# Another order for the first loads, scans and splits of a gated scan feeding two feed-forward layers

## The reference

```
sig = 1 / (1 + exp(-f_logit));  f = lb + (1 - lb) * sig;  i = 1 - f
h = f[:, t] * h + i[:, t] * x[:, t];  y[:, t] = h          # t = 0 .. 6079
x1 = g1(y @ w_in0) @ w_out0       # g1(h) = h * sigmoid(1.702 * h)
z  = g2(x1 @ w_in1) @ w_out1      # g2(h) = 0 below -1, h above 1, (h + 1)^2 / 4 between
```

## Time and profile before

| | |
|---|---|
| median of three runs | 1020.7 us |
| the profiled execution | 1021.38 us |
| its span, first to last instruction | 1019.6 us |
| PE busy | 1009.2 us, 99% of the span |
| DVE, ACT, POOL busy | 67%, 69%, 57% |
| mean granted clock of PE, share of full | 0.998 |
| DMA | 130.76 MB, mean 128 GB/s; 277 and 235 GB/s in the first two slices of 25.5 us |

### The profile page before, as it was taken

The page is one execution under the profiler, slowest core; times in us unless marked ns, Lnnn a source line. Parts: engine busy times, 40 slices in busy tenths (PEclk is TensorE's granted clock), DMA queues, the critical chain, the costliest instruction groups (busy, mean ns, idle before and its releaser), DMA issues.

```text
span 1019.6 us, 14153 instructions
## 1 busy us (share of the span) xinstructions
PE 1009.2 (99%) x4401; PEld 823.6 (81%) x4401; DVE 686.8 (67%) x958; ACT 705.2 (69%) x1306; POOL 579.6 (57%) x471
## 2 busy tenths in 40 slices
PE   7999999999999999999999999999999999999998
PEld 5988988888888888888888888888888888888886
DVE  5864867675676786666678666668665456767676
ACT  6666767666676677667677676767766667777665
POOL 3567768757577465356636436645635664573432
PEclk9999999999999999999999999999999999999999
DMA  7776574435622222442322334232323223232421
GB/s 277 235 232 223 183 250 160 166 114 205 207 106 99 83 83 99 155 150 73 107 74 95 135 114 144 73 109 72 109 74 131 91 75 107 73 109 73 146 76 42
DMA packets 53212, 130.76 MB, mean 128 GB/s; under 512 B 6032, under 2 KB 16912, under 8 KB 52112
## 3 DMA queue, kind: packets, MB, share of 16 engines
q1 hardware_dynamic: 52992, 129.59, 36.5%
q10 hardware_dynamic: 144, 0.26, 0.1%
HBM read 106.82 MB, written 23.00 MB: 127 GB/s over the span
## 4 chain that ended last, share of the span: by engine, by line
PE 97%; ACT 1%; POOL 1%; DMA 0%; DVE 0%; issue 0%; SPq 0%; POOLq 0%; ACTq 0%
PE chain L561 26%; PE acc L616 17%; PE acc L613 17%; PE acc L612 17%; PE pair L561 13%; PE single L561 7%; DMA gate<-f_logit_dram 0%; POOL xin1lo L1415 0%; ACT g_hi L908 0%; DVE xin0lo L1143 0%; POOL w_main L1378 0%; SPq L489 0%; POOL g_lo L1441 0%; ACT g_act L894 0%; ACT xin0hi L795 0%
## 5 line engine op out<-in xcount | busy, mean ns | idle before, releaser
L1441 POOL TENSOR_TENSOR g_lo<-g_act,g_hi 128x512 fp32r<-128x512 f32 (+1 forms) x269 | 354.3, 1318 | 395.9 <-ACT g_hi L908 391.2
L868 ACT ACTIVATE spare<-chain 128x512 f32<-128x512 f32 x240 | 143.3, 597 | 189.8 <-PE chain L561 189.2
L1198 DVE TENSOR_TENSOR spare<-pair,spare 128x512 f32<-128x512 f32 x160 | 110.5, 691 | 182.3 <-PE pair L561 181.8
L908 ACT ACTIVATE g_hi<-g_act 128x512 fp32r<-128x512 f32 (+1 forms) x269 | 168.1, 625 | 5.5 <-DVE g_act L1222 3.4
L561 PE MATMUL chain<-xin1hi,w_main 128*128 128x512 f32 x416 | 162.5, 395 | 0.0
L616 PE MATMUL acc<-g_lo,w_down0hi 128*128 128x512 f32 (+1 forms) x384 | 150.3, 391 | 0.0
L612 PE MATMUL acc<-g_hi,w_down0hi 128*128 128x512 f32 (+1 forms) x384 | 149.8, 390 | 0.3 <-ACT g_hi L908 0.3
L616 PE MATMUL acc<-g_lo,w_down1hi 128*128 128x512 f32 (+1 forms) x384 | 150.1, 391 | 0.0
L613 PE MATMUL acc<-g_hi,w_down1lo 128*128 128x512 f32 (+1 forms) x384 | 150.0, 391 | 0.0
L613 PE MATMUL acc<-g_hi,w_down0lo 128*128 128x512 f32 (+1 forms) x384 | 150.0, 391 | 0.0
L612 PE MATMUL acc<-g_hi,w_down1hi 128*128 128x512 f32 (+1 forms) x384 | 149.7, 390 | 0.0
(11 more groups left out here) (125 smaller groups left out, 1966.1 us busy)
## 6 DMA issues: line engine op xcount, KB each, us to landing
w_main<-sums_kept SPq DMA_DIRECT2D x80, 512.0 KB, 3.6
w_main<-blocks_kept SPq DMA_DIRECT2D x80, 256.0 KB, 2.9
w_a<-blocks_kept SPq DMA_DIRECT2D x80, 128.0 KB, 3.9
blocks_kept<-w_main SPq DMA_DIRECT2D x16, 512.0 KB, 4.3
w_main<-blocks_kept SPq DMA_DIRECT2D x16, 512.0 KB, 3.4
sums_kept<-xin0hi SPq DMA_DIRECT2D x16, 512.0 KB, 2.9
zout<-w_in_dram SPq DMA_DIRECT2D x23, 256.0 KB, 4.3
out_dram<-zout SPq DMA_DIRECT2D x10, 512.0 KB, 5.5
```

Source lines behind the costliest of these rows:

```text
L868: act.activation(snap[k][:, 0:n], chain[g % 2][:, 0:n], ACT.Copy).then_inc(s_snap, 1)
L908: act.activation(g_hi[h % 4][:, 0:n], activated(h), ACT.Copy).then_inc(s_ghi, 1)
L1198: dve.tensor_tensor(to[:, 0:n], bank[:, 0:n], snap[(0, 2, 1)[k]][:, 0:n], ALU.add).then_inc(s_evac, 1)
L1441: pool.tensor_tensor(g_lo[h % 4][:, 0:n], g_act[h % 4][:, 0:n], g_hi[h % 4][:, 0:n].bitcast(F32), ALU.subtract).then_inc(s_glo_pool, 1)
```

## The change

- **First loads (SP and ACT).** The bound `lb` (1 KB) is issued by ACT and block 0 of the weights by SP. SP's order becomes gate part 0, gate part 1, first half of x, block 0, second half of the gate, block 1, second half of x; the rest stays.
- **Order on ACT.** `first_hi(0)` stands ahead of `sigmoid_step(0, 2)`; `first_hi(1)` ahead of `blocks_hi(0, 1)`; `f_step(0, 2)` behind both; `first_hi(2)` and `first_hi(3)` ahead of both `down_hi`.
- **Order on DVE.** Drive and scan of parts 0 and 1 run one after the other, then remainders 0 and 1; drive and scan of parts 2 and 3, then remainder 3.
- **One remainder on POOL.** Remainder 2 is made by POOL, after `blocks_lo(0, 1)` and ahead of `down_lo(0, 0)`. PE and SP wait for it on a semaphore of its own.
- **Next inputs.** `x_lo(1, 0)` moves from step 13 to step 11 of stage 0, waiting for `down_lo(0, 6)` instead of `down_lo(0, 7)`; `x_lo(1, 1)` moves from step 14 to 13 and waits for `down_lo(0, 7)`.

The number of matmuls, of compute instructions and of bytes moved stays the same.

```diff
-            load_first(gate, f_logit, part_columns(0, 0)[0], s_gate_first[0])
-            sp.dma_start(lb[:], lower_bound).then_inc(s_lb, 16)
+            for q in range(K):
+                load_first(gate, f_logit, part_columns(0, q)[0], s_gate_first[q])
             load_first(state, x, half(0), s_x_first[0])
-            load_first(gate, f_logit, part_columns(0, 1)[0], s_gate_first[1])
+            load_raw_up(0, 0)
+            load_first(gate, f_logit, half(1), s_gate_early[1])
             load_raw_up(0, 1)
-            load_first(gate, f_logit, half(1), s_gate_early[1])
             load_first(state, x, half(1), s_x_first[1])
...
                     for k in range(K):
-                        pe.wait_ge(s_first_lo, 2 * h + k + 1)
+                        if (h, k) == (1, 0):
+                            pe.wait_ge(s_first_lo_pool, 1)
+                        else:
+                            pe.wait_ge(s_first_lo, h + k + 1)
...
-            act.dma_start(raw_up[0], up_source[0][0]).then_inc(s_raw_up[0], 16)
+            act.dma_start(lb[:], lower_bound).then_inc(s_lb, 16)
             sigmoid_step(0, 0)
             sigmoid_step(0, 1)
             blocks_hi(0, 0)
+            first_hi(0)
             sigmoid_step(0, 2)
-            first_hi(0)
+            first_hi(1)
+            blocks_hi(0, 1)
             f_step(0, 2)
-            blocks_hi(0, 1)
-            first_hi(1)
             sigmoid_step(0, 3)
             f_step(0, 3)
             first_hi(2)
+            first_hi(3)
             down_hi(0, 0)
-            first_hi(3)
             down_hi(0, 1)
...
-            drive_step(0, 0)
-            scan_step(0, 0)
-            drive_step(0, 1)
+            for q in range(2):
+                drive_step(0, q)
+                scan_step(0, q)
             first_lo(0)
-            scan_step(0, 1)
-            drive_step(0, 2)
             first_lo(1)
-            scan_step(0, 2)
-            drive_step(0, 3)
-            first_lo(2)
-            scan_step(0, 3)
+            for q in range(2, 4):
+                drive_step(0, q)
+                scan_step(0, q)
             first_lo(3)
...
+            def first_lo(q):
+                cols, k, _ = part_columns(0, q)
+                at = first_columns(q)
+                pool.wait_ge(s_first_hi, q + 1)
+                pool.tensor_tensor(xin[0][1][:, k, at], state[:, cols], xin[0][0][:, k, at].bitcast(F32),
+                                   ALU.subtract).then_inc(s_first_lo_pool, 1)
+
...
                 if si == 0:
-                    if s == 13:
-                        pool.wait_ge(s_down_dve, down_made(0, NG - 1)[1])
-                    if s in (13, 14):
-                        x_lo(1, s - 13)
+                    if s in (11, 13):
+                        pool.wait_ge(s_down_dve, down_made(0, s // 2 + 1)[1])
+                        x_lo(1, s // 13)
...
             blocks_lo(0, 1)
-            pool.wait_ge(s_first_lo, 4)
+            first_lo(2)
+            pool.wait_ge(s_first_lo, 3)
             down_lo(0, 0)
```

More of the change, by code:

```diff
@@ L265, in build @@
         s_scan, s_carry = sem("s_scan"), sem("s_carry")
-        s_first_hi, s_first_lo = sem("s_first_hi"), sem("s_first_lo")
+        s_first_hi, s_first_lo, s_first_lo_pool = sem("s_first_hi"), sem("s_first_lo"), sem("s_first_lo_pool")
         s_direct_hi, s_direct_lo = sem("s_direct_hi"), sem("s_direct_lo")
@@ L399, in load_third @@
                 if t == 0:
-                    sp.wait_ge(s_first_lo, 4)
+                    sp.wait_ge(s_first_lo, 3)
+                    sp.wait_ge(s_first_lo_pool, 1)
                 else:
```

## The result

| | before | changed kernel |
|---|---|---|
| median (us), beside each other | 1021.79 | 1018.53 |
| lowest to highest of 9 runs each | 1019.45 to 1023.07 | 1017.95 to 1019.20 |
| the profiled execution | 1021.38 | 1018.12 |
| its span | 1019.6 | 1016.3 |

The ratio is 0.9971, with a 95% interval of 0.9960 to 0.9981: 0.29% faster, and the near end of the interval lies at 0.19%. The forecast was 1017.5 with a range of 1016.0 to 1020.0. The runs of before have a higher median here (1021.79) than the three that the prediction knew (1020.7).

A forecast was written before the change was run, and what follows sets the result against it. PE was taken to bound the kernel (97% of the span), so only its waits and lower-clock stretches, nearly all in the first 20 us, counted. 3.3 + 0.25 = 3.55 us gave 1017.15, taken as 1017.5; range 1016.0 to 1020.0.

The forecast's parts named there:

- Landing times by KB: First loads: landing times read off by KB asked for; block 0 at 5.8 us, bounds 4.8 and 6.7.
- Remainder 0 beside POOL: Before the first product: DVE's remainder waits for POOL, ends about 8.1; PE starts at 8.15 us instead of 9.12.
- The wait for block 1's weights: In the up products: PE waits 0.4 us for block 1 and goes on at 9.9 us.
- The clock: Up products from 11.09 us: the half clock after two idle gaps goes away, worth 1.75 us.
- the rival: At the start: the clock falls anyway, 1.75 us come back, 1019.2 us; chance 0.15.
- What is late next: After the up products: down product at 14.4, store of block 0 lands 14.8, tile 4 at 16.15; gain 3.3 us.
- Next inputs: Before stage 1: earlier remainders remove the 0.45 us wait at 49.08; 0.25 us gained, bounds -0.35 and 0.45.
- Sum: Whole kernel: 3.3 + 0.25 = 3.55 us gained, giving 1017.15 from the median of 1020.7; taken as 1017.5.
- The slow rival: Middle of stage 0: block 4's store does not move, PE loses 2.9 us plus 1.75 of clock, 1021.8; chance 0.05.

The follow-up runs named there:

- bridged: store_first with ten warming matmuls instead of nine and one more after block 0's weights are ready; median 1017.47 us, ratio 0.9964 against before.
- eleven: store_first with eleven warming matmuls in a row instead of nine; median 1018.60 us, ratio 0.9968 against before.
- loads_only: The kernel before with only the new order of first loads and the bound on ACT's queue; median 1018.83 us, ratio 0.9977 against before.
- order_only: The changed kernel with the old loads and old places of the next inputs' remainders; median 1020.13 us, ratio 0.9990 against before.
- gaps_filled: The kernel before with six more matmuls on the constant, two before the first product, four in the second gap; median 1019.75 us, ratio 0.9985.
- split_late: The changed kernel with the next inputs' two remainders back at their old steps; median 1019.03 us, ratio 0.9976 against before.
- remainder_dve: The changed kernel with remainder 2 back on DVE, between scan 2 and drive 3; median 1019.20 us, ratio 0.9978 against before.
- store_first_again: store_first unchanged, measured a second time beside the changed kernel; median 1018.37 us, ratio 0.9969 against before.
- store_first: The changed kernel with the store of block 0 issued ahead of the next chunk's gate and x loads; median 1017.57 us, ratio 0.9963 against before.
- store_late: The changed kernel with two more down-weight loads issued before the store of block 0; median 1019.93 us, ratio 0.9986 against before.
- after_again: The changed kernel as it is, measured a second time; median 1018.37 us, ratio 0.9968 against before.

## Why the prediction was right, point by point

**Landing times by KB.** Block 0 was taken at 5.8, and came at 5.37 (5.27 in bridged, 6.24 in eleven, with the same loads ahead of it). The second gate part came early as said: ACT took it at 3.67 (3.5 forecast). The first product is 0.4 us ahead of the forecast (7.75 against 8.15), since ACT took block 0 0.48 sooner than the 5.85 of the working. The bounds of block 0 were added up slightly low: an issue near 2.1 and 2.9 or 4.7 us give 5.0 and 6.8, not 4.8 and 6.7. It took 3.2 us.

**Remainder 0 beside POOL.** It takes 1.10 at 6.51, while POOL works on block 0 from 6.09, as forecast; 1.08 in loads_only beside POOL, 0.39 in order_only with POOL idle. Beside POOL the remainder ends 0.27, 0.24 and 0.26 us after POOL's instruction does (before, loads_only, changed), so it waited for the end of that and was not merely slowed down. By the lock between DVE and GpSimd, in which the one that comes second waits for the other's whole instruction (the Trainium skill, SBUF — State Buffer, Who interferes with whom), it should be so, and all three agree.

**The wait for block 1's weights.** Forecast 9.5 to 9.9; it was between 9.04 and 9.49, and cost about a quarter of a microsecond instead of 0.4. POOL's remainder 2 ran 9.99 to 10.66, 0.67 against an estimate of 0.6.

**The clock.** Not lost again: the forecast held in the profiled executions of the changed kernel, and gaps_filled has no half rate either. The term was mis-sized by 0.3: 1.42 us for 1.75, since the sum counted 42 matmuls at 0.111 each (4.66 us) for the full clock, and in gaps_filled they took about 5.0 (10.74 to 15.62, and one more). The earlier start made good for it: the up products ended near 13.6, for 13.9 in the forecast. What else was wrong is the form of the rival. It was taken as a fall after the gaps; in four of the profiles here (order_only, split_late, remainder_dve, store_first_again) it was a rise that came only at about 12 to 13 us, at a cost of the same size. The Trainium skill (TensorE: Matmul & The Clock Gate, What's actually happening) says that the moment differs from run to run, and store_first and store_first_again agree: from first product to first down product 6.14 us in one and 7.74 in the other, 1.60 apart. The section gives the moment a spread of half a microsecond either way; here it is larger, with the full rate from 7.74 on in one and from about 12 in the other. In the changed kernel a late rise is partly hidden: PE is ready for tile 4 at about 15.7 and held until 16.3 anyhow. No profile of the changed kernel itself shows one, but split_late has the same start, instruction for instruction, and had a late rise: from first product to tile 4 it took 9.41 us, for 8.53 in the changed kernel, so 0.88 more and not 1.60. That fits the changed kernel's runs, 1.25 us from lowest to highest over 9, where before had 3.6.

**What is late next.** Down product forecast 14.4, seen 14.03; ACT held by the store until 14.8, seen 14.82; tile 4 forecast 16.15, seen 16.28; gain there 3.3, seen 3.17. The 0.1 is the step from ACT's start to PE's, 1.46 for 1.35: with ACT held, the slack in the 1.74 us of before came out as 0.28, not 0.4. This was the step that mattered: without the cap the sum would have been 0.25 or more too high.

**Next inputs.** This term was mis-sized. 0.25 us was to come on top of 3.3 at stage 1, and the wait did go. But between tile 4 and stage 1 the changed kernel takes 29.67 us, the kernel before 29.64, and order_only, gaps_filled, store_first, remainder_dve and four more 29.38 to 29.41. Before, the surplus is the gap at 49.08, as in split_late (29.70). In the changed kernel it stands at the beginning: PE's second product of unit 1 waits until 18.15 for POOL's remainder of the activation, which itself came late because ACT's row is late behind the store (loads_only, store_late and after_again, in which ACT also starts 1.50 us or less ahead of tile 4, have 29.66 to 29.70 too):

```profile
16.95 1.15 POOL L1449 TENSOR_TENSOR g_lo<-g_act,g_hi 128x448 fp32r<-128x448 f32 x1 [2.76 <-ACT g_hi L912]
```

It ends at 18.10. So a wait of 0.25 left and one of about the same size came, at another place: the store's wait costs more than the arrival of tile 4 shows.

**Sum.** 3.55 was forecast from the profiled execution, 3.26 came (1021.38 to 1018.12): 0.1 at tile 4, the rest the term above. The forecast of 1017.5 was further set by the median of three; 1018.53 is 1.0 above it. Some of that is the median of before, which was 1020.7 over three runs and 1021.79 over nine. That the median fell below the 1018.65 which the prediction drew for "faster" is a near thing: 4 of the 9 runs lie above it.

**The slow rival** did not come. ACT waited for the store of block 4 until 33.23 (2.00 us), which was 36.59 before: the store moved with all else, by 3.36, and PE has no idle time there. Block 7's remainder, which the new places push back, ran from 38.92 to 40.22, and tile 14 started at 41.06 without a wait: cost nought, as forecast.

## What to carry to other kernels

In a kernel whose first microseconds are bound by loads, read what a landed block releases as a chain of turns (who splits it, who takes its remainder, whose store frees it), and put the store that frees a buffer ahead of loads that are needed later: here that store was the cap, worth 0.9 us in a profiled start with an early clock. Gaps in PE of a microsecond at the start may cost a second time through the clock, so price them with the lower rate and ask whether a later wait hides that. And before the second decimal of a saving is believed, run the same kernel twice: two executions of one program differed by 1.7 us at tile 4.

store_first and bridged are the best found, at ratios of 0.9963 and 0.9964 in one comparison each, against 0.9971 and 0.9968 of the changed kernel; taken with store_first_again (0.9969) the intervals overlap throughout, so that they beat it is what the profiles suggest (tile 4 at 15.4 to 15.9 when the clock is up early), not something the times show.

## What the runs showed of the hardware that was not expected

- The clock's rise from 1.2 to 2.4 GHz came at one of two times: during the warming or by just after the first product, or only at about 12 to 13 us. The late one is in four of the eight profiles in which the nine warming matmuls took 4.00 us, and in none of the three in which they took 3.50 to 3.85. The idle time after the warming does not tell them apart: after_again had 0.51 us and the full rate from the first product at 7.86, store_first_again 0.50 and remainder_dve 0.52 and the half rate until 12. What decides is open.
- In the record the granted clock reads 1.00 ahead of its first change, while 6 or 7 matmuls per us go through, the same as at 0.50.
- Over a gap of 0.97 us up to 9.53, after one of 0.18, the clock did not fall (loads_only); in the kernel before it fell after two gaps of 1.07 and 1.08, and in store_late after gaps of 1.16 and 0.43.
- Block 0, a load of 256 KB with the same loads ahead of it, landed anywhere from 5.2 (loads_only) to 6.2 us (eleven) between executions, over half as wide as the bounds that the prediction gave it (4.8 to 6.7).
